# First tile by plain two-bank products, weight sums spread over that tile, first loads on one queue: a gated scan with a squared-ReLU layer, one Trainium2 core

## What is computed

```python
# x, f_logit (2, 6080, 256); lower_bound (256,); w_in (256, 2048); w_out (2048, 256)
f = lower_bound + (1 - lower_bound) * sigmoid(f_logit)
for t in range(S):
    h = f[:, t] * h + (1 - f[:, t]) * x[:, t]
    y[:, t] = h
out = relu(y @ w_in) ** 2 @ w_out
```

## Time and profile before

| | |
|---|---|
| median of 3 runs | 1014.37 us (1013.77 to 1015.68) |
| profiled execution, own time | 1014.93 us |
| its span, first to last instruction | 1012.8 us |
| TensorE busy | 990.8 us (98%) |
| VectorE busy | 755.4 us (75%) |
| ScalarE busy | 698.8 us (69%) |
| GpSimd busy | 60.2 us (6%) |
| mean granted TensorE clock | 0.993 |

### The profile page before, as it was taken

One profiled execution on the slowest core, in us unless ns is written; L12 is line 12 of the kernel. 1 busy time (PEld: TensorE's weight loads), 2 busy tenths in 40 slices (PEclk: granted clock), 3 DMA queues, 4 the chain that ended last, 5 costly groups with the idle time before them and its releaser, 6 DMA issues.

```text
span 1012.8 us, 12625 instructions
## 1 busy us (share of the span) xinstructions
PE 990.8 (98%) x4348; PEld 815.2 (80%) x4348; DVE 755.4 (75%) x966; ACT 698.8 (69%) x942; POOL 60.2 (6%) x63
## 2 busy tenths in 40 slices
PE   6889999999999999999999999999999999999998
PEld 3777888888888888888888888888888888888886
DVE  7799787688687687778768768767867877876545
ACT  4766776776676676677677667667767677766664
POOL 5674000000000000000000000000000000000000
PEclk7999999999999999999999999999999999999999
DMA  3501201201100110210120110111021012000001
GB/s 135 188 1 42 79 1 41 84 1 42 63 22 20 64 42 0 83 42 0 41 84 0 41 62 21 41 43 42 0 83 42 0 48 78 1 1 23 21 1 42
DMA packets 22046, 42.07 MB, mean 42 GB/s; under 512 B 1520, under 2 KB 3056, under 8 KB 22000
## 3 DMA queue, kind: packets, MB, share of 16 engines
q1 hardware_dynamic: 21536, 40.83, 11.7%
q10 hardware_dynamic: 432, 0.72, 0.2%
q0 software_dynamic: 32, 0.00, 0.0%
HBM read 29.10 MB, written 12.45 MB: 41 GB/s over the span
## 4 chain that ended last, share of the span: by engine, by line
PE 90%; DVE 6%; issue 2%; ACT 1%; POOL 0%; DVEq 0%; ACTq 0%
PE out_ps L703 48%; PE hidden_ps L688 42%; DVE g_lo L492 1%; DVE x_in L407 1%; DVE x_in L398 1%; DVE f_in L418 1%; DVE g_hi L487 1%; DVE h L574 0%; DVE f_in L387 0%; DVE h L554 0%; DVE sums_lo L451 0%; ACT p L284 0%; DVE plain_lo L461 0%; DVE plain_hi L459 0%; POOL wc_lo L650 0%
## 5 line engine op out<-in xcount | busy, mean ns | idle before, releaser
L703 PE MATMUL out_ps<-g_hi,w_out_hi 128*128 128x512 f32 (+1 forms) x768 | 298.5, 389 | 5.6 <-DVE g_lo L492 5.5
L703 PE MATMUL out_ps<-g_lo,w_out_hi 128*128 128x512 f32 (+1 forms) x768 | 297.5, 387 | 0.0
L703 PE MATMUL out_ps<-g_hi,w_out_lo 128*128 128x512 f32 (+1 forms) x768 | 297.5, 387 | 0.0
L492 DVE TENSOR_TENSOR g_lo<-h,g_hi 128x1024 fp32r<-128x1024 f32 (+1 forms) x191 | 237.3, 1242 | 62.1 <-ACT g_hi L302 58.8
L703 PEld LDWEIGHTS out_ps<-g_hi,w_out_hi 128*128 128x128 f32 x768 | 144.3, 188 | 38.2 <-issue 5.9
L703 PEld LDWEIGHTS out_ps<-g_hi,w_out_lo 128*128 128x128 f32 x768 | 144.3, 188 | 28.4
L703 PEld LDWEIGHTS out_ps<-g_lo,w_out_hi 128*128 128x128 f32 x768 | 144.3, 188 | 28.4
L688 PE MATMUL hidden_ps<-sums_hi,wc_hi 128*128 128x512 f32 (+1 forms) x384 | 150.6, 392 | 3.7 <-POOL wc_lo L650 2.6
L688 PE MATMUL hidden_ps<-sums_lo,wc_hi 128*128 128x512 f32 (+1 forms) x384 | 149.9, 390 | 1.8 <-DVE sums_lo L451 1.8
L688 PE MATMUL hidden_ps<-sums_hi,wc_lo 128*128 128x512 f32 (+1 forms) x384 | 149.5, 389 | 0.0
L574 DVE TENSOR_TENSOR h<-hidden_ps,u 128x512 f32<-128x512 f32 (+1 forms) x96 | 65.8, 686 | 90.3 <-PE hidden_ps L688 90.2
(11 more groups left out here) (58 smaller groups left out, 1043.7 us busy)
## 6 DMA issues: line engine op xcount, KB each, us to landing
x_in<-x_t SPq DMA_DIRECT2D x22, 512.0 KB, 4.5
f_in<-f_logit_t SPq DMA_DIRECT2D x22, 512.0 KB, 4.7
out_t<-result SPq DMA_DIRECT2D x21, 512.0 KB, 3.1
w_out_raw<-w_out_t SPq DMA_DIRECT2D x8, 256.0 KB, 8.1
w_in_raw<-w_in_t SPq DMA_DIRECT2D x7, 256.0 KB, 8.3
f_in<-f_logit_t SPq DMA_DIRECT2D x4, 224.0 KB, 4.6
out_t<-result SPq DMA_DIRECT2D x2, 448.0 KB, 3.0
out_t<-result SPq DMA_DIRECT2D x2, 256.0 KB, 2.2
```

The costliest lines, as they stand in the source:

```text
L492: nc.vector.tensor_tensor(g_lo[b][:, :, 0:n], h[b][:, :, 0:n], g_hi[b][:, :, 0:n].bitcast(F32), ALU.subtract).then_inc(g_ready[b], 1)
L703: mm = nc.tensor.matmul(out_ps[:, b, c, 0:n], half[:, j, m, c * P:(c + 1) * P], moving[b][:, m, 0:n], start=(j == 0 and m == 0 and k == 0) ...
```

## The change

The first tile no longer uses the seven products. Its eight plain products are made for one sequence at a time (a pair): two banks of PSUM, 12 matmuls, one ReLU that reads both banks, one square. The fourth weight block A21 is split too and kept in the slot of `S2` until pair 1 of its quad is done; only then do ScalarE and GpSimd put the halves of the sums there, so the sums of quad j - 1 are made in quad j, and those of quad 7 in tile 1, which is the first to read them. T sums of the narrow y aren't made any more. VectorE splits w_out alone (`split_w_out`). The y blocks' low halves are made by GpSimd for sequence 0 and VectorE for sequence 1. `bound` is loaded by ScalarE's queue, and all first loads of f, x and weights by SP's, in order f00, x00, f01, x01, f10, x10, f11, w_in 0, x11, w_in 1. Loads of tile 1 wait for the narrow y alone. The dummy matmuls are 34 at the start and none later. The tiles from 1 on keep their seven products; there ScalarE's second ReLU of a quad carries the semaphore that the square waits for.

```diff
@@ constants and memory @@
-WARM_UP = 16
-KEEP_WARM = 6
+WARM_UP = 34
...
+A21 = S2
...
+            w_out_raw = sb("w_out_raw", [P, QUADS, 2, C * P], within=early)
             w_in_raw = sb("w_in_raw", [P, QUADS, 4, P], within=early)
-            w_out_raw = sb("w_out_raw", [P, QUADS, 2, C * P], within=early)
@@ blocks of the first tile @@
+        def first_block(plain, sums, b, c):
+
+            return sums[0][:, 0, 0:NARROW] if (b, c) == (1, 0) else plain[0][:, b + c, 0:NARROW]
@@ SP: loads @@
+            def load_first(b, c):
                 sp.dma_start(f_in[:, b, c, 0:NARROW], f_logit[b, :, c, tokens(0)]).then_inc(first_f[b][c], 16)
+                if (b, c) == (1, 1):
+                    load_w_in(0)
                 sp.dma_start(x_in[:, b, c, 0:NARROW], x[b, :, c, tokens(0)]).then_inc(first_x[b][c], 16)
...
+                sp.wait_ge(state_done, 4 * it)
                 if isinstance(it, int) and it == 1:
-                    for v in (B11, B21, B22):
-                        sp.wait_ge(first_ready[v], 1)
+                    for b in range(B):
+                        for c in range(C):
+                            sp.wait_ge(first_ready[b][c], 1)
                 else:
                     sp.wait_ge(y_ready, y_count(it - 1, 3))
-                sp.wait_ge(t_done, 4 * it)
-                sp.wait_ge(state_done, 4 * it)
+                    sp.wait_ge(t_done, 4 * (it - 1))
...
-            load_first_f(0, 0)
-            load_first_f(0, 1)
-            load_first_f(1, 0)
-            load_first_x(1, 0)
-            load_first_f(1, 1)
-            load_first_x(1, 1)
+            for b in range(B):
+                for c in range(C):
+                    load_first(b, c)
             load_w_in(1)
@@ ScalarE @@
+            def first_relu(j, b):
+                act.wait_ge(pair_done[b], j + 1)
+                if j > 0:
+                    act.wait_ge(g_ready[b], j)
+                nc.scalar.activation(h[b][:, :, 0:NARROW], hidden_ps[:, 2 * b:2 * b + 2, 0:NARROW], ACT.Relu
+                                     ).then_inc(relu_done[b], 1)
+
+            def first_quad(j):
+                first_relu(j, 0)
+                square_pair(0, j, 0)
+                if j + 2 < QUADS:
+                    plain_w_in_hi(j + 2)
+                if 1 <= j <= B * C:
+                    gate(1, (j - 1) // C, (j - 1) % C)
+                if j > 0:
+                    sum_w_in_hi(j - 1)
+                first_relu(j, 1)
+                square_pair(0, j, 1)
+                hi_pair1(0, j)
...
-            for c in range(C):
-                act.dma_start(x_in[:, 0, c, 0:NARROW], x[0, :, c, tokens(0)]).then_inc(first_x[0][c], 16)
-            act.dma_start(w_in_raw[:, 0], w_in[:, 0]).then_inc(w_in_loaded[0], 16)
+            act.dma_start(bound[:], lower_bound).then_inc(bound_loaded, 16)
@@ VectorE @@
-            def round_w_out(q):
+            def split_w_out(q):
                 dve.wait_ge(w_out_loaded[q], 16)
                 nc.vector.tensor_copy(w_out_hi[:, q], w_out_raw[:, q]).then_inc(w_out_hi_done, 1)
+                dve.wait_ge(w_out_hi_done, q + 1)
+                nc.vector.tensor_tensor(w_out_lo[:, q], w_out_raw[:, q], w_out_hi[:, q].bitcast(F32), ALU.subtract
+                                        ).then_inc(w_out_ready, 1)
...
+            def first_quad(j):
+                if j > 0:
+                    lo_pair(0, j - 1, 1)
+                ahead(1, 1, j - 1)
+                hi_pair0(0, j)
+                lo_pair(0, j, 0)
+                ahead_late(1, 1, j - 1)
+                if j + 1 < QUADS:
+                    split_w_out(j + 1)
+                else:
+                    ahead(1, 1, 7)
...
-            first_plain_lo(B21, 0, 1)
-            t1(0)
-            input_part(0, 1, 1)
-            scan_part(0, 1, 1)
-            t2(0)
-            first_sum_lo(0)
-            t3(0)
-            first_sum_lo(1)
-            t4(0)
-            first_sum_lo(2)
-            first_sum_lo(3)
-            first_plain_lo(B22, 1, 1)
+            for b in range(B):
+                for c in range(C):
+                    input_part(0, b, c)
+                    scan_part(0, b, c)
+            for c in range(C):
+                first_y_lo(1, c)
@@ GpSimd @@
-            pool.dma_start(bound[:], lower_bound).then_inc(bound_loaded, 16)
...
+            for c in range(C):
+                first_y_lo(0, c)
+            plain_w_in_lo(0)
             for q in range(QUADS):
-                plain_w_in_lo(q)
+                if q + 1 < QUADS:
+                    plain_w_in_lo(q + 1)
                 w_in_sums(q)
                 if q > 0:
-                    rest_of_w_out(q - 1)
-                sum_w_in_lo(q)
-            rest_of_w_out(QUADS - 1)
+                    sum_w_in_lo(q - 1)
+            sum_w_in_lo(QUADS - 1)
@@ TensorE @@
+            def first_pair(j, b, passes):
+
+                if j > 0:
+                    pe.wait_ge(relu_done[b], j)
+                for k, (half, of) in enumerate(passes):
+                    for m, blocks in enumerate(((A11, A12), (A21, A22))):
+                        for c in range(C):
+                            if j == 0:
+                                pe.wait_ge(first_hi[b][c] if of is hi_of else first_ready[b][c], 1)
+                            if b == 0:
+                                pe.wait_ge(w_plain_ready if half is wc_lo else w_plain_hi_done, j + 1)
+                            mm = nc.tensor.matmul(hidden_ps[:, 2 * b + m, 0:NARROW], half[:, j, blocks[c]],
+                                                  first_block(*of, b, c), start=(k == 0 and c == 0),
+                                                  stop=(k == 2 and c == C - 1), skip_group_check=True)
+                mm.then_inc(pair_done[b], 1)
...
+            def first_quad(j):
+                first_pair(j, 0, ((wc_hi, hi_of), (wc_hi, lo_of), (wc_lo, hi_of)))
+                if j > 0:
                     for m in range(2):
                         for c in range(C):
-                            second(it, 0, 1, m, c)
+                            second(0, j - 1, 0, m, c)
+                first_pair(j, 1, ((wc_hi, hi_of), (wc_lo, hi_of), (wc_hi, lo_of)))
+                if j > 0:
+                    for m in range(2):
+                        for c in range(C):
+                            second(0, j - 1, 1, m, c)
```

More of the change, by code:

```diff
@@ L142, in program, with run @@
         block = ctx.enter_context(nc.Block())
-        def run(eng, quad):
-            for s in range(2 * QUADS):
-                quad(s // QUADS, s // QUADS, s % QUADS)
+        def run(eng, first_quad, quad):
+            for j in range(QUADS):
+                first_quad(j)
+            for j in range(QUADS):
+                quad(1, 1, j)
             with eng.Fori(1, IT // 2 - 1) as k:
@@ L798, in _ @@
+                product3(it, odd, j)
+                if very_last(it, j):
+                    second(*prev, 1, 0, 0)
+                second(*prev, 1, 0, 1)
+                second(*prev, 1, 1, 0)
+                second(*prev, 1, 1, 1)
             pe.wait_ge(zeros_done, 1)
-            keep_warm(WARM_UP)
-            run(pe, quad)
+            for _ in range(WARM_UP):
+                nc.tensor.matmul(out_ps[:, 1, 1], zeros[:, 0:P], zeros[:], start=True, stop=True)
+            run(pe, first_quad, quad)
```

318 lines of the change are left out of this document (121 added, 197 removed).

## The result

| | before | after |
|---|---|---|
| median of the runs | 1014.07 us (4 runs) | 996.8 us (996.74 to 996.89, 4 runs) |
| ratio | | 0.9827 [0.981, 0.9844] |
| profiled execution, span | 1012.8 us | 994.7 us |
| first full-width product | 104.20 us | 87.91 us |
| from there to the end of the span | 908.6 us | 906.8 us |

The kernel is 17.3 us faster; the forecast was 998.3 us in a range of 996.0 to 1003.0. The gain has two parts, and only the first was forecast: 16.3 us lie in the first tile, and 1.8 us behind it.

The account below looks back on a forecast made before the run. First tile bound by its start, then VectorE; TensorE alone after. Pair 1's end 18.5 + low clock 1.6 + seven quads 68.0 = 88.1 us against 104.2, 16.1 less: 998.3 us, range 996.0 to 1003.0.

Parts of the forecast that it names:

- main term: First tile: TensorE as the limit takes 68.0 us for seven quads, 9.72 us each.
- the forecast's 59.5 to 70.7: First tile: VectorE's need for seven quads, 46.2 us undisturbed plus 1.9 to 3.5 us a quad lost to GpSimd.
- Rival (b): First tile: VectorE and GpSimd set it by the lock, seven quads 70.7 us instead of 68, 1001.0 us; chance 14%.
- The first forget: Start: with bound on ScalarE's queue and f alone ahead, it starts at 4.2 us instead of 6.01.
- the other reckoning: Start: by the skill's first-byte latency of the sync/scalar path alone, the first forget would move by 0.4 us.
- the last scan: Start: VectorE's last scan ends at 15.6 us, 11.2 us after the first forget, less 1.6, plus 1.8 for GpSimd.
- TensorE's first pair runs from about 11.2: Start: the first pair begins at about 11.2 us, after the cast of w_in 0, and ends at 14.0.
- I expect one such stretch after these 2.3 idle us: Start: after TensorE's wait in pair 1, 3.4 us of work at half clock, costing 1.6 us.
- rival (a): Start: the clock doesn't fall, 1.6 us less, 996.7 us; chance 22%.
- No wait of the second-layer matmuls for g_lo: First tile: a sign of the forecast, that TensorE's second-layer matmuls never wait for g_lo.
- The 3.7 us of slack: First-tile quad: 7.3 us of matmuls cover a chain of 3.6 us, so VectorE may come 3.7 us late.
- From tile 1 on the 908.6 us of before: Behind the first tile: same work, so unchanged at 908.6 us from the first full-width product on.

Follow-up runs that it names:

- experiment 6: Changed kernel with one more VectorE subtraction in each quad of the first tile; 998.65 us, ratio 0.9844.
- experiment 7: Changed kernel with two more VectorE subtractions in each quad of the first tile; 1003.84 us, ratio 0.9887.
- Experiment 8: Changed kernel with the low half of w_out back on GpSimd, behind the plain low halves of the next weights; 999.11 us, ratio 0.9841.
- Experiment 10: Changed kernel with the first x block on ScalarE's queue behind bound, and the f blocks first on SP's queue; 997.92 us, ratio 0.9837.
- Experiment 12: Changed kernel with first x on ScalarE's queue, f first on SP's, plus eight keep-warm matmuls between the first two pairs; 996.21 us, ratio 0.9818.
- experiment 5: Changed kernel with 16 dummy matmuls at the start instead of 34; 997.38 us, ratio 0.9824.
- experiment 1: Changed kernel with 80 more instructions of already fulfilled waits on ScalarE ahead of its loop over tiles; 1000.08 us, ratio 0.9849.
- experiment 2: Kernel before with 80 already fulfilled waits on ScalarE in the first tile, 40 more instructions before the loop; 1012.93 us, ratio 0.9978.
- experiment 3: Kernel before with only the change's new order and queues of the first loads; 1015.42 us, ratio 1.0001.
- experiment 9: Changed kernel with the first loads on SP's queue reordered: f00, f01, x00, x10 after f10, f11, weights, x11 last; 998.15 us, ratio 0.9835.
- experiment 4: Changed kernel with the order and queues of the first loads of the kernel before; 998.77 us, ratio 0.9845.

## Why the prediction was right, and where it wasn't

**The time and its main term held.** From the end of pair 1 (18.41) to the first full-width product are 69.50 us: 1.33 more than the usual spacing at the first `g_lo`, and 68.17 for seven quads, forecast 68.0. TensorE is the only limit from 22 us on; experiments 6 and 7 put VectorE's reserve between one and two extra subtractions, 0.7 to 1.4 us of the forecast's undisturbed time a quad. By that estimate its need for seven quads was 58 to 63 us, at the low end of the forecast's 59.5 to 70.7 or just below it. Rival (b) was one extra subtraction and a bit away. Experiment 8 speaks for w_out's low half on VectorE: on GpSimd the profiled execution is 3.1 us longer, but 1.6 of that is the low clock, and the intervals of the two ratios overlap.

**The start: right sum, two terms wrong.** The first forget (4.14 for 4.2; `bound` landed 2.9 us after its issue on ScalarE's queue against 4.4 on GpSimd's, so the forget moved by 1.9 us and not by the 0.4 of the other reckoning), the last scan (15.29 for 15.6) and the end of pair 1 (18.41 for 18.5) came as forecast. "TensorE's first pair runs from about 11.2" failed: it was 12.61. I had looked only at the first f; the second, third on the queue, landed at 6.07 and held up gate, scan and the cast of w_in 0, which stands behind them. So TensorE's idle time lay ahead of pair 0 (1.54 us) and not inside pair 1, where I had 2.3.

**"I expect one such stretch after these 2.3 idle us" failed.** No low clock came: 1.6 us less, rival (a)'s outcome, but not after the stop that it spoke of. Experiment 10 is nearly the forecast's own case: first product at 11.12 (11.2), `plain_hi` at 16.25 (16.3), then the low clock, pair 1 done at 20.15 (20.1), first full-width product at 88.25 (88.1). Experiment 12 shows the cost of that clock by taking it away: 1.5 us at the end of pair 1 (forecast 1.6), 1.1 behind the wait for `g_lo`. The price was about right, but the stop that it needs was not there, and by experiment 5 the wait for `g_lo` would have hidden most of it.

**"No wait of the second-layer matmuls for g_lo" failed once.** The 3.7 us of slack were reckoned with VectorE free. In quad 0 it isn't: from 15.2 to 22.0 us it works without a pause at low halves, state, split of w_out, `g_hi` and `g_lo`, the last at 2.06 us beside GpSimd instead of 1.09. That cost 1.33 us. With -0.1 for pair 1, -1.6 for the clock, +1.33 here and +0.17 for the quads the sum is -0.2, the 87.91 for 88.1. That this number came so near is luck: two errors cancelled.

**"From tile 1 on the 908.6 us of before" failed by 1.8 us**, and this is the whole miss of the profiled execution (996.9 for 998.8). I took the same work for the same time and asked of each edit only which data it makes late. Experiments 1 and 2 show the cause: ScalarE's code for the first tile became shorter and moved its loop, and with the old place went a wait for instructions at each of three jumps back. That the place was a better one is chance.

## What to carry to other kernels

Where a loop costs the same few tenths at each turn and the profile blames "issue", look at the instruction queue: the place of the loop in an engine's code is part of a change's price, and a few dozen harmless instructions show it. An earlier load is worth only what stands directly behind it on the slowest chain; experiment 3 moved the first product by 1.6 us and the end of its first tile by 0.2, and experiments 9 and 10 got their f sooner and lost it to VectorE and to a low clock. A busy share of 98% doesn't tell a limit from a full but patient engine; add a known amount of work and look at the engine that waits.

## What of the hardware was unexpected

A stop of TensorE doesn't by its length alone decide on the clock: 1.81 us were followed by 0.51 in experiment 10 and by a full clock in experiment 4; 1.96 us (8) by the low level and 1.98 us (6) by a full clock; 1.83 us (9) and 2.89 us (7) by the low level, and in the changed kernel 1.54 and 1.16 us by none. Nor does the kernel decide: of the four executions of experiment 4 one has a mean clock of 1.0 and three have 0.998, and of experiment 10 likewise. What makes the difference is open here. Eight matmuls on zeros in the stop held the clock (12). The spacing of 448-wide matmuls has two values at full clock. It is 0.2067 us throughout the first tile in experiments 1, 5 and 9, 0.2027 in the changed kernel and most others of its kind (in the kernel before the means of stretches lie between the two), and in experiment 6 it goes from the one to the other at the short wait near 76 us; the busy time of one reads 368 ns in the first case and 365 in the second. From 100 us on, 512 wide, it is 0.227 in all. What sets it is open; an error of 1.3 us lies in it for any forecast of such a tile. Instructions came in packets of 8 KB on the queue that goes with the gaps of ScalarE's loop, 26 from 110 to 1000 us before and 10 from 90 to 985 after.
